# Weight splits by casting DMAs and GpSimd, the normalisation and the gate's low product on VectorE, tokens evacuated before the gate

## The reference

```python
scores = (q @ k.T) / 8 + bias            # 2 batches, 8 heads, 768 positions, head size 64
a = exp(scores - max); a = a / (sum(a) + 1e-9); x = a @ v      # masked to window and globals
h = x @ w_in                             # 512 -> 2048
P = a0 + a1*h + a2*h**2 + a3*h**3
Q = 1 + |b0|*|h| + |b1|*h**2
x = (P / (Q + 1e-6)) @ w_out             # 2048 -> 512
h = x @ w2_in                            # 512 -> 1024
solu = h * softmax(h); ln = (solu - mean) / sqrt(var + 1e-6) * g_ln
out = ln @ w2_out                        # 1024 -> 512
```

## Time and profile before

| | us |
|---|---|
| median of 3 runs | 516.46 (515.97 to 517.37) |
| the profiled execution | 517.32 |
| its span, first to last instruction | 515.5 |
| TensorE busy | 499.6 (97%) |
| VectorE busy | 366.1 (71%) |
| ScalarE busy | 289.4 (56%) |
| GpSimd busy | 124.0 (24%) |
| attention, first transposes to the last units' values | 10.5 to 105.7 |
| start to start of two 128x512 matmuls, at full clock / half clock | 0.227 / 0.427 |

### The profile page before, as it was taken

One profiled execution on the slowest core, in us unless ns is written; L12 is line 12 of the kernel. 1 busy time (PEld: TensorE's weight loads), 2 busy tenths in 40 slices (PEclk: granted clock), 3 DMA queues, 4 the chain that ended last, 5 costly groups with the idle time before them and its releaser, 6 DMA issues.

```text
span 515.5 us, 7169 instructions
## 1 busy us (share of the span) xinstructions
PE 499.6 (97%) x2572; PEld 392.6 (76%) x2572; DVE 366.1 (71%) x689; ACT 289.4 (56%) x502; POOL 124.0 (24%) x133
## 2 busy tenths in 40 slices
PE   6999999987999999899999989999999999999997
PEld 5665555766888888788888868888888888888885
DVE  5579898279999987777756888887875555555540
ACT  4799989565566555554545666556444344334441
POOL 3456666304322232111132222234300000000000
PEclk9799999997999999999999999999999999999999
DMA  8676548100000000000001122311111221211101
GB/s 302 234 290 237 192 162 326 58 3 0 1 0 1 1 1 0 1 0 0 1 0 42 51 83 86 110 41 41 42 41 54 69 62 61 61 61 61 61 28 54
DMA packets 24079, 37.64 MB, mean 73 GB/s; under 512 B 1904, under 2 KB 16240, under 8 KB 23024
## 3 DMA queue, kind: packets, MB, share of 16 engines
q1 hardware_dynamic: 23760, 37.23, 21.0%
q10 hardware_dynamic: 288, 0.01, 0.0%
HBM read 27.79 MB, written 3.15 MB: 60 GB/s over the span
## 4 chain that ended last, share of the span: by engine, by line
PE 90%; DVE 4%; ACT 2%; issue 2%; POOL 1%; DMA 1%; DVEq 0%
PE ps L1030 9%; PE ps L1031 9%; PE ps L1032 9%; PE ps L970 8%; PE ps L971 8%; PE ps L972 8%; PE ps L916 5%; PE ps L906 4%; PE ps L1093 4%; PE ps L1095 4%; PE ps L1050 4%; PE ps L1094 4%; PE ps L1048 4%; PE ps L1049 4%; PE ps L931 4%; PE ps L1076 2%
## 5 line engine op out<-in xcount | busy, mean ns | idle before, releaser
L392 POOL TENSOR_TENSOR gate_lo<-rest,recq 128x1024 fp32r<-128x1024 f32 x24 | 71.2, 2968 | 204.9 <-DVE rest L758 204.9
L1030 PE MATMUL ps<-gate_hi,bank_b_hi 128*128 128x512 f32 x192 | 76.0, 396 | 8.3 <-issue 5.0
L737 DVE SCALAR_TENSOR_TENSOR quad<-quad,small,absh 128x1024 f32<-128x1024 f32 x24 | 44.8, 1868 | 49.9 <-ACT absh L450 49.9
L1031 PE MATMUL ps<-gate_lo,bank_b_hi 128*128 128x512 f32 x192 | 75.7, 394 | 0.0
L1032 PE MATMUL ps<-gate_hi,bank_b_lo 128*128 128x512 f32 x192 | 75.5, 393 | 0.0
L970 PE MATMUL ps<-tok_hi,bank_a_hi 128*128 128x512 f32 x192 | 75.2, 392 | 0.0
L971 PE MATMUL ps<-tok_lo,bank_a_hi 128*128 128x512 f32 x192 | 74.8, 390 | 0.0
L972 PE MATMUL ps<-tok_hi,bank_a_lo 128*128 128x512 f32 x192 | 74.7, 389 | 0.0
L388 POOL TENSOR_SCALAR probs<-probs,small 128x256 f32<-128x256 f32 (+1 forms) x96 | 50.5, 537 | 42.4 <-DVE small L629 42.4
L447 ACT ACTIVATE quad<-ps 128x1024 f32<-128x1024 f32 x24 | 24.7, 1028 | 52.4 <-DVE rest L755 52.4
L409 ACT ACTIVATE probs<-negs,small 128x256 f32<-128x256 f32 (+1 forms) x96 | 46.4, 485 | 8.4 <-DVE small L619 6.7
(11 more groups left out here) (93 smaller groups left out, 996.4 us busy)
## 6 DMA issues: line engine op xcount, KB each, us to landing
v_sb<-in_v_win SPq DMA_DIRECT2D x8, 704.0 KB, 4.2
bank_a_raw<-in_w_in SPq DMA_DIRECT2D x4, 1024.0 KB, 8.4
bank_b_raw<-in_w_out SPq DMA_DIRECT2D x4, 1024.0 KB, 9.7
q_sb<-in_q_t SPq DMA_DIRECT2D x16, 192.0 KB, 3.8
k_sb<-in_k_win SPq DMA_DIRECT2D x8, 384.0 KB, 4.8
stage_hi<-tok_hi SPq DMA_DIRECT2D x12, 256.0 KB, 2.7
stage_lo<-tok_lo SPq DMA_DIRECT2D x12, 256.0 KB, 2.8
out_dram<-out_sb SPq DMA_DIRECT2D x12, 256.0 KB, 2.0
```

What stands on the lines that cost most here:

```text
L392: pool.tensor_tensor(gate_lo[g % 2][:], rest[g % 2][:], recq[:], ALU.mult).then_inc(gate_lo_ready, 1)
L737: dve.scalar_tensor_tensor(quad[:], quad[:], abs_b1, absh[par][:], ALU.mult, ALU.add).then_inc(quad_ready, 1)
L1030: pe.matmul(banks(4 + k, 1), bank_b_hi[:, f, ws], g_hi, start=first, stop=False)
L1031: pe.matmul(banks(4 + k, 1), bank_b_hi[:, f, ws], g_lo, start=False, stop=False)
```

## The change

- The normalisation moves from GpSimd to VectorE, at the head of `attend_unit`.
- The high parts of all weights come by casting DMAs from the weights in memory, issued by GpSimd: w_in in four of 1 MB from unit 2 on, every third unit; w_out in eight of 512 KB, once the last heads are copied out; the second feed-forward's in eight of 512 KB, as up tiles free bank_a.
- w_in's low parts move from VectorE to GpSimd, one every second unit from unit 14.
- gate_lo moves from GpSimd to VectorE.
- `mid_high` and `mid_low` stand ahead of `gate_reciprocal` and `gate_quotient`.

```diff
-    SPLIT_FROM = 12
+    SPLIT_FROM, CAST_FROM = 14, 2
...
+        def cast_w_in(i):
+            tiles = slice(4 * i, 4 * i + 4)
+            pool.dma_start(bank_a_hi[:, tiles, :], w_in[:, tiles]).then_inc(in_hi_loaded[i], 16)
+
+        def split_in_low(f):
+            if f % 4 == 0:
+                pool.wait_ge(in_loaded[f // 4], 16)
+                pool.wait_ge(in_hi_loaded[f // 4], 16)
+            pool.tensor_tensor(bank_a_lo[:, f, :], bank_a_raw[:, f, :], bank_a_hi[:, f, :].bitcast(F32),
+                               ALU.subtract).then_inc(in_lo_ready, 1)
+
         with pool.If(take == 1):
             for n in range(HEADS):
-                pbuf, lo = n % PB, 0 if n % BLOCKS else P
-                pool.wait_ge(dve_step, n * STEPS_PER_BLOCK + SETUP_STEPS + 2)
-                for h in range(2):
-                    pv = probs[pbuf][:, h, lo:WIN]
-                    pool.tensor_scalar(pv, pv, prec[pbuf][:, h:h + 1], 1.0, ALU.mult, ALU.mult).then_inc(probs_ready, 1)
-
-        for g in range(N_GROUPS):
-            pool.wait_ge(rest_ready, g + 1)
-            pool.tensor_tensor(gate_lo[g % 2][:], rest[g % 2][:], recq[:], ALU.mult).then_inc(gate_lo_ready, 1)
+                pool.wait_ge(scores_ready, n + 1)
+                i, part = divmod(n - CAST_FROM, 3)
+                if part == 0 and 0 <= i < 4:
+                    cast_w_in(i)
+                f, part = divmod(n - SPLIT_FROM, 2)
+                if part == 0 and 0 <= f < FT:
+                    split_in_low(f)
+        with pool.Else():
+            for i in range(4):
+                cast_w_in(i)
+            for f in range(FT):
+                split_in_low(f)
+
+        pool.wait_ge(heads_hi, HEADS)
+        for j in range(FT // 2):
+            tiles = slice(2 * j, 2 * j + 2)
+            pool.dma_start(bank_b_hi[:, tiles, :], w_out[:, tiles]).then_inc(outw_hi_loaded[j], 16)
+
+        for j in range(FT // 2):
+            tiles = slice(2 * j, 2 * j + 2)
+            src = w2_in[:, tiles] if j < FT // 4 else w2_out[:, 2 * j - FT // 2:2 * j - FT // 2 + 2]
+            pool.wait_ge(hidden_ready, (CHUNKS - 1) * FT + 2 * j + 2)
+            pool.dma_start(bank_a_hi[:, tiles, :], src).then_inc(w2_hi_loaded[j], 16)
...
-        def high_parts(bank_hi, bank_raw, j, done):
-            act.activation(bank_hi[:, 2 * j:2 * j + 2, :], bank_raw[:, 2 * j:2 * j + 2, :], ACT.Copy).then_inc(done, 1)
...
-            else:
-                act.wait_ge(heads_lo, HEADS)
-                act.wait_ge(outw_loaded[0], 16)
-                high_parts(bank_b_hi, bank_b_raw, 0, outw_hi_ready)
-            gate_reciprocal(g)
-            if c == 0 and j + 1 < GROUPS:
-                act.wait_ge(outw_loaded[(j + 1) // 2], 16)
-                high_parts(bank_b_hi, bank_b_raw, j + 1, outw_hi_ready)
-            elif c == CHUNKS - 1:
-                for s in (2 * j, 2 * j + 1):
-                    act.wait_ge(w2_loaded[s], 16)
-                high_parts(bank_a_hi, bank_a_raw, j, w2_hi_ready)
             if c and j == 1:
                 mid_high(c - 1)
+            gate_reciprocal(g)
...
-        def split_in_high(f):
-            if f % 4 == 0:
-                dve.wait_ge(in_loaded[f // 4], 16)
-            dve.tensor_copy(bank_a_hi[:, f, :], bank_a_raw[:, f, :]).then_inc(in_hi_ready, 1)
-
-        def split_in_low(f):
-            dve.wait_ge(in_hi_ready, f + 1)
-            dve.tensor_tensor(bank_a_lo[:, f, :], bank_a_raw[:, f, :], bank_a_hi[:, f, :].bitcast(F32),
-                              ALU.subtract).then_inc(in_lo_ready, 1)
+        def attend_norm(n):
+
+            pbuf, lo = n % PB, 0 if n % BLOCKS else P
+            dve.wait_ge(dve_step, n * STEPS_PER_BLOCK + (SETUP_STEPS + 2))
+            for h in range(2):
+                pv = probs[pbuf][:, h, lo:WIN]
+                dve.tensor_scalar(pv, pv, prec[pbuf][:, h:h + 1], None, ALU.mult).then_inc(probs_ready, 1)
 
         def attend_unit(n):
 
+            attend_norm(n)
...
-            f, part = divmod(n - SPLIT_FROM, 2)
-            if 0 <= f < FT:
-                (split_in_low if part else split_in_high)(f)
...
+            dve.wait_ge(rest_ready, g + 1)
+            dve.tensor_tensor(gate_lo[par][:], rest[par][:], recq[:], ALU.mult).then_inc(gate_lo_ready, 1)
+
+        def low_parts(bank_hi, bank_lo, bank_raw, j, done):
             tiles = slice(2 * j, 2 * j + 2)
-            dve.wait_ge(*made_hi)
...
+        def split_out_low(j):
+            dve.wait_ge(outw_loaded[j // 2], 16)
+            dve.wait_ge(outw_hi_loaded[j], 16)
+            low_parts(bank_b_hi, bank_b_lo, bank_b_raw, j, outw_lo_ready)
+
         for g in range(N_GROUPS):
             c, j = divmod(g, GROUPS)
             if g:
                 gate_poly(g)
             else:
-                low_parts(bank_b_hi, bank_b_lo, bank_b_raw, 0, (outw_hi_ready, 1), outw_lo_ready)
-            gate_quotient(g)
+                split_out_low(0)
             if c and j == 1:
                 mid_low(c - 1)
+            gate_quotient(g)
             gate_rest(g)
             if c == 0 and j + 1 < GROUPS:
-                low_parts(bank_b_hi, bank_b_lo, bank_b_raw, j + 1, (outw_hi_ready, j + 2), outw_lo_ready)
+                split_out_low(j + 1)
             elif c == CHUNKS - 1:
-                low_parts(bank_a_hi, bank_a_lo, bank_a_raw, j, (w2_hi_ready, j + 1), w2_lo_ready)
+                for s in (2 * j, 2 * j + 1):
+                    dve.wait_ge(w2_loaded[s], 16)
+                dve.wait_ge(w2_hi_loaded[j], 16)
+                low_parts(bank_a_hi, bank_a_lo, bank_a_raw, j, w2_lo_ready)
```

More of the change, by code:

```diff
@@ L200, in attention_feed_forwards @@
     w2_loaded = [sem(f"w2_loaded{i}") for i in range(FT)]
-    in_hi_ready, in_lo_ready, outw_hi_ready, outw_lo_ready = (sem("in_hi_ready"), sem("in_lo_ready"),
-                                                              sem("outw_hi_ready"), sem("outw_lo_ready"))
-    w2_hi_ready, w2_lo_ready = sem("w2_hi_ready"), sem("w2_lo_ready")
+    in_hi_loaded = [sem(f"in_hi_loaded{i}") for i in range(4)]
+    outw_hi_loaded = [sem(f"outw_hi_loaded{i}") for i in range(FT // 2)]
+    w2_hi_loaded = [sem(f"w2_hi_loaded{i}") for i in range(FT // 2)]
+    in_lo_ready, outw_lo_ready, w2_lo_ready = sem("in_lo_ready"), sem("outw_lo_ready"), sem("w2_lo_ready")
     hidden_ready, act_in_ready, quad_ready, poly_ready = sem("hidden_ready"), sem("act_in_ready"), sem("quad_ready"), sem("poly_ready")
@@ L759, in gate_rest @@
                                      ALU.subtract).then_inc(rest_ready, 1)
-        def low_parts(bank_hi, bank_lo, bank_raw, j, made_hi, done):
+            dve.wait_ge(rest_ready, g + 1)
+            dve.tensor_tensor(gate_lo[par][:], rest[par][:], recq[:], ALU.mult).then_inc(gate_lo_ready, 1)
+        def low_parts(bank_hi, bank_lo, bank_raw, j, done):
             tiles = slice(2 * j, 2 * j + 2)
-            dve.wait_ge(*made_hi)
             dve.tensor_tensor(bank_lo[:, tiles, :], bank_raw[:, tiles, :], bank_hi[:, tiles, :].bitcast(F32),
@@ L785, in _ @@
             full_attention()
-            for f in range(FT):
-                split_in_high(f)
-                split_in_low(f)
             gate_poly(0)
```

## The result

The changed kernel takes 523.51 us (median of 4 executions, 521.32 to 524.06) against 516.22 (515.95 to 517.37) of the kernel before beside it: ratio 1.0121, 95% interval 1.0083 to 1.0160, so slower by 1.2% (the two medians alone give 1.4%, inside the interval). The forecast was 518.5 with a range up to 523.0. The sign was right. The time stands at the upper end of the range: 0.5 us above it by the median, 0.3 inside it if the ratio is put on the 516.46 from which the range was built (522.7). The profiled execution took 524.06 with a span of 522.2.

What follows compares the result with a forecast made beforehand. TensorE, busy 97%, was taken as the bound, with VectorE left no cover in attention. Terms +9.0 - 2.1 - 2.4 - 2.5 = +2.0 took the profiled 517.3 to 519.3, or 518.5 against the median 516.46; range 508.5 to 523.

Steps and rivals of the forecast that it cites:

- The sign: Whole kernel: predicted slower, +2.0 us in sum; slower was given a chance of 0.54.
- Attention, +9.0: Attention units 14 to 44: GpSimd's w_in products hold VectorE, +9.0 us, bounds -3.3 and +14.5.
- no cover is left: Attention: without waits VectorE needs 20.1 us per twelve units against TensorE's 20.4, so every VectorE wait is paid.
- the base: Attention: twelve units without product stalls put at 20.1 us, summed from VectorE's start distances.
- it takes the port as the shift starts: Attention: product starts with VectorE's shift (0.35 us), so the sums behind wait the rest of 1.20, 0.85.
- w_in's casts, 0: Attention, units 2 to 11: 4 MB more of casting DMAs, costed at 0, at most 9.7 us.
- Seam, -2.1: Seam to first feed-forward: first w_out cast takes 4.2 us, TensorE restarts at 117.0 against 119.21, -2.1 us.
- The clock, -2.4: Behind the seam: a 2.9 us stop leaves the clock up, twelve matmuls at 0.227 instead of 0.427, -2.4 us.
- rival 3: Seam: the clock falls all the same, as the stop is 2.9 against 3.2; 520.9 us, chance 0.20.
- Gate's low product, 0 in the groups; quad 1.28: Chunk 0 groups: gate_lo adds 1.21 us on VectorE, quad falls from 2.69 to 1.28; cost 0.
- Borders, -2.5: Two chunk borders: low tokens come sooner without gate_hi ahead, waits fall to some 0.3 each, together -2.5 us.
- Rival 1's point that decides: Attention: below 0.72 us of stall per product the whole is faster; rival 1 (508.5 us) had chance 0.20.

Runs made afterwards that it cites:

- e1: Changed kernel with w_in's low products on GpSimd cut from 512 to 8 columns and w_in's raw loads cast by GpSimd's queue: 513.53 us, ratio 0.9940.
- e4: Changed kernel with each GpSimd product made to wait until unit n-1 is normalised: 519.58 us, ratio 1.0077.
- e6: e2 with w_out's first low part behind gate_lo instead of ahead of gate_hi: 508.92 us, ratio 0.9842.
- e7: e6 with w_in's four casts issued at units 8, 16, 24 and 32 instead of 2, 5, 8 and 11: 507.48 us, ratio 0.9804.
- e3: Changed kernel with each 128x512 GpSimd product split in four of 128 columns: 513.71 us, ratio 0.9953.
- e8: Kernel before with only the gate's low product moved from GpSimd to VectorE: 512.51 us, ratio 0.9940.
- e5: Kernel before with only the tokens' evacuation moved ahead at the two chunk borders: 513.65 us, ratio 0.9930.
- e2: Changed kernel with the normalisation back on GpSimd and w_in's low parts back on VectorE: 513.08 us, ratio 0.9937.
- e10: Changed kernel with the edits of e3 and e7 together (quartered products, casts spread, w_out's first low part behind gate_lo): 510.75 us, ratio 0.9887.
- e9: Kernel before with the edits of e5 and e8, w_out's first high and low parts behind the gate's operations, no casting DMA: 505.65 us, ratio 0.9797.
- e11: The kernel of e7 run again, beside e9 on one chip: 508.29 us, ratio 0.9846.

## Why the prediction was right, and where it was off

**Attention, +9.0 against +11.0: the mis-sized term.** The mechanism, and its place in units 14 to 44, are as put: a product holds VectorE, and "no cover is left". Its size, 0.85, is measured as 0.85 by the stretched groups and 0.78 by e1's pace, but that agreement is in part luck: it was worked out for sums behind a shift (1.20 less 0.35), and of the 13.6 us measured the sums have 0.6 and the normalisations 13.1. What was low is the base: twelve units without products were put at 20.1 from VectorE's start distances "without any wait", and e1 shows 21.10. The distances themselves hold (a full unit runs from 35.53 to 37.05, 1.52 for 1.51). Left out were TensorE's own least time, 20.4 by the same prediction, and VectorE's waits for ScalarE's exponentials: in e1 1.3 us of those twelve units. So 21.10 + 6 x 0.78 = 25.77 stands against the 25.2 forecast, +4.1 per twelve units for +3.5, which makes +9.4 between units 12 and 42 and +1.7 behind them, where two more products fall. The step "it takes the port as the shift starts" failed: when the scores that release a product are done, VectorE is still at the normalisation of an earlier unit, so that is the victim, and not the sums. e4, with the sums as victim, shows that the price is the same (0.86). The rule of the Trainium skill that speaks of this, page "SBUF — State Buffer", section "Who interferes with whom", has GpSimd and VectorE exclude each other for shared-port operations; the trace agrees, down to a 128x2 instruction that took 1.25 us.

**w_in's casts, 0.** Right in the changed kernel: no wait for a load shows. e6 and e7 agree; e3 and e4, with the same casts, had one wait for k_sb each (3.1 and 1.4), so the cover isn't safe.

**Seam, -2.1 against -2.0.** The first cast landed in 4.08 us for the 4.2 taken. Every distance after it is as summed. What the step didn't ask is why the low part must stand ahead of gate_hi; e6 shows that this order cost 2 us and made the stop long enough to matter.

**The clock, -2.4 against 0.** This step failed in the profiled execution. It argued that a stop of 2.9 us is shorter than the 3.2 after which the clock had fallen, but in the changed kernel it fell 2.3 us after the stop began. In e1, e3 and e8 it stayed up through 2.90, 2.87 and 2.92; in e4 it fell in a stop of 2.84. In these five traces the length of the stop doesn't tell whether the clock falls. From restart to border 1 the changed kernel took 90.37 and e1 87.55, both with a border wait of 0.23: the fall costs 2.8 us, for 2.3 by the same reckoning in the kernel before (91.20, less 1.32 of longer wait at the border). The term is therefore +0.5. The one execution of the changed kernel at 521.32, 2.7 under the profiled one, may be one in which it stayed up; there is no trace of it, and its mean clock, 0.993, is also that of the one at 523.16. In rival 3 the fall stood with 0.20.

**Gate's low product, 0 in the groups; quad 1.28.** Right: 1283 ns, and no wait in chunk 0. e8 shows what it is worth alone: 3.5 us by the medians (its interval allows 1.3 to 4.9), 2.1 of it by the trace in the shorter stop, the rest where the clock stays up behind it.

**Borders, -2.5 against -2.8.** Waits of 1.55 and 1.73 became 0.23 each: 2.8. e5 alone gives 2.4.

With the clock (+0.5 for -2.4), the attention (+2.0), the seam (+0.1) and the borders (-0.3), 519.3 becomes 524.0; the profiled execution took 524.06.

Rival 1's point that decides, 0.72 us of stall per product, did decide: the changed kernel is above it with 0.85, e3 with 0.31 is below and faster than before. With e1's base and the 4.3 us that seam and borders really gave, the point itself lies lower, at about 0.4 (an estimate: 21.10 + 6s = 21.71 + 12/31 x 4.3); both kernels stay on their sides of it.

**Where the gain went.** The change holds four parts. Two pay, the gate's low product (3.5) and the borders (2.4). The casts pay nothing: ScalarE had the time, and at the seam the cast (4.08 us to landing) is slower than ScalarE's copy (two in 1.99). The exchange of normalisation and products between VectorE and GpSimd costs some 10 us (523.51 to e2's 513.08).

## What to carry to other kernels

Before work goes to GpSimd next to a loaded VectorE, look whether it is one long SBUF instruction: here it shut out whatever VectorE did next from SBUF, however small, and the cost was the meeting, not the load. Short instructions, or long ones on VectorE itself, cost less, but look in the trace whether VectorE does get in between the short ones. At a seam between stages, list what each instruction ahead of the first matmul reads, and put what waits for a late transfer behind what doesn't. Price a part by itself before a bundle is judged: here two good parts were hidden under one bad one, and a third was worth nothing.

## What the runs showed of the hardware

- A GpSimd product of 128x512 (1.27 us) held VectorE's 128x2 tensor_scalar for 1.25 us (0.17 alone). Four of 128x128 (0.465 each) held it 0.31 in all on average (e3), though they are 1.86 us of GpSimd time: VectorE mostly gets in between them. In e10 it didn't at two of the three products that stand right behind the issue of a cast, and was held for 1.25 and 1.13.
- A shift, which reads PSUM, isn't held: in the changed kernel one starts at 37.58 and takes its 0.42 us beside a product from 37.65 to 38.92.
- The clock fell 3.2 us after TensorE had stopped in the kernel before, 2.3 in the changed one and 2.0 in e4; after e2's stop of 3.30 it fell only behind the restart, as it did behind the waits for k_sb of 3.23 (e1) and 3.07 (e3), and after three stops of 2.87 to 2.92 not at all. A stop of 1.05 us never brought it down in a profiled execution (e6, e7, e9, e10, e11). A short stop at the seam doesn't make the times steady by itself: e9's executions lie within 1.6 us of each other, but e11's, with the same stop, within 4.4, where e8's lie within 4.7. The clock is lost elsewhere too: between 10 and 20 us it was 0.66 in the kernel before and in the changed one, and 1.00 in e4.
- A casting DMA of 512 KB behind an idle queue was waited for by VectorE until 4.08 us after its issue (3.9 to 4.4 in e1 to e4); the median of the eight was 6.6, that of the four 1 MB casts 8.7.
